# Three chained blocks in one kernel: new orders in the head and the first two stages, and the last block turned in groups of 96 tokens

## The reference

```python
def _attn_ref(q, k, v, g_norm):                 # [8, 8, 576, 64]
    kv = np.einsum('bhsd,bhse->bhde', k, v)
    out = np.einsum('bhsd,bhde->bhse', q, kv)
    rms = np.sqrt(np.mean(out * out, axis=-1, keepdims=True) + 1e-06)
    return out / rms * g_norm
# x = out as [4608, 512]
x = sigmoid(x @ w_gate) * (x @ w_val) @ w_out          # d_ff = 1536
x = silu(x @ w2_gate) * (x @ w2_val) @ w2_out
```

## Time and profile before

| what | us |
|---|---|
| median of 3 runs | 1748.52 (1748.45 to 1750.14) |
| the profiled execution | 1748.58 |
| its span, first to last instruction | 1745.8 |
| TensorE busy | 1721.4 (99%) |
| VectorE, ScalarE, GpSimd busy | 1205.7, 905.0, 377.6 |

### The profile page before, as it was taken

The page is one execution under the profiler, slowest core; times in us unless marked ns, Lnnn a source line. Parts: engine busy times, 40 slices in busy tenths (PEclk is TensorE's granted clock), DMA queues, the critical chain, the costliest instruction groups (busy, mean ns, idle before and its releaser), DMA issues.

```text
span 1745.8 us, 30864 instructions
## 1 busy us (share of the span) xinstructions
PE 1721.4 (99%) x11182; PEld 1689.5 (97%) x11182; DVE 1205.7 (69%) x1937; ACT 905.0 (52%) x1772; POOL 377.6 (22%) x326
## 2 busy tenths in 40 slices
PE   9999999999999999999999999999999999999998
PEld 7899899999999999999998999999999999999998
DVE  4977677787666678666679877787666668655555
ACT  5776676555444445444456555565444445444444
POOL 4722222013111125111126000013111125111111
PEclk9999999999999999999999999999999999999999
DMA  8786776576555566555555555566555566555553
GB/s 235 239 276 201 262 260 218 213 281 243 199 200 199 199 219 248 195 201 200 195 186 206 198 200 199 199 246 240 201 197 201 195 227 237 167 176 189 185 183 91
DMA packets 168982, 366.91 MB, mean 210 GB/s; under 512 B 12672, under 2 KB 128896, under 8 KB 168832
## 3 DMA queue, kind: packets, MB, share of 16 engines
q1 hardware_dynamic: 168832, 364.96, 61.1%
HBM read 234.36 MB, written 130.55 MB: 209 GB/s over the span
## 4 chain that ended last, share of the span: by engine, by line
PE 80%; DVE 2%; POOL 1%; issue 1%; ACT 0%; DVEq 0%; ACTq 0%; POOLq 0%
PE ps L833 78%; PE ps L775 1%; DVE arena L1398 0%; POOL arena L1650 0%; DVE arena L1380 0%; DVE wa L1236 0%; DVE hop L1330 0%; PE ps L694 0%; POOL wops L1595 0%; POOL wops L1594 0%; PE ps L674 0%; POOL wops L1592 0%; PE ps L707 0%; PE ps L681 0%; POOL wops L1597 0%
## 5 line engine op out<-in xcount | busy, mean ns | idle before, releaser
L833 PE MATMUL ps<-xo,wa 128*128 128x384 f32 x6048 | 1077.9, 336 | 6.2 <-ACT arena L1032 3.2
L833 PEld LDWEIGHTS ps<-xo,wa 128*128 128x128 f32 x6048 | 1047.3, 188 | 10.3 <-issue 4.0
L1032 ACT ACTIVATE arena<-ps 128x384 f32<-128x384 f32 x648 | 316.9, 491 | 566.9 <-PE ps L833 564.7
L1380 DVE TENSOR_TENSOR arena<-ps,arena 128x384 f32<-128x384 f32 x648 | 352.6, 553 | 361.6 <-PE ps L833 284.2
L833 PE MATMUL ps<-hop,wb 128*128 128x384 f32 x3024 | 538.1, 335 | 1.0 <-DVE arena L1398 0.7
L833 PEld LDWEIGHTS ps<-hop,wb 128*128 128x128 f32 x3024 | 522.9, 188 | 4.9 <-issue 1.7
L1650 POOL TENSOR_TENSOR arena<-arena 128x384 f32<-128x384 f32 x144 | 147.5, 1049 | 734.3 <-DVE arena L1380 734.3
L1330 DVE TENSOR_TENSOR hop<-arena,hop 128x384 fp32r<-128x384 f32 (+1 forms) x396 | 276.0, 719 | 34.1 <-ACT hop L1014 27.9
L1014 ACT ACTIVATE hop<-arena 128x384 fp32r<-128x384 f32 (+1 forms) x396 | 233.3, 609 | 63.4 <-DVE arena L1398 34.3
L1046 ACT ACTIVATE arena<-arena 128x384 f32<-128x384 f32 x216 | 112.7, 522 | 64.8 <-DVE arena L1380 64.7
L1398 DVE TENSOR_TENSOR arena<-arena 128x384 f32<-128x384 f32 x216 | 128.7, 597 | 20.3 <-DVE arena L1380 1.4
(11 more groups left out here) (76 smaller groups left out, 796.0 us busy)
## 6 DMA issues: line engine op xcount, KB each, us to landing
xo<-x_operands SPq DMA_DIRECT2D x168, 768.0 KB, 6.2
x_operands<-xo SPq DMA_DIRECT2D x84, 768.0 KB, 5.1
x<-arena SPq DMA_DIRECT2D x120, 384.0 KB, 3.2
arena<-x SPq DMA_DIRECT2D x96, 384.0 KB, 4.6
xraw<-x SPq DMA_DIRECT2D x22, 768.0 KB, 6.5
wops<-in_moe_w_gate_dram SPq DMA_DIRECT2D x24, 256.0 KB, 4.8
wops<-in_moe_w_val_dram SPq DMA_DIRECT2D x24, 256.0 KB, 4.2
wops<-in_moe_w_out_dram SPq DMA_DIRECT2D x48, 128.0 KB, 2.3
```

The source lines that it names most:

```text
L833: mm = pe.matmul(dst, lhsT, rhs, start=(pr in (1, 5, 2) and c == 0 and i == 0), stop=(c == 1 and i == 2), skip_group_check=(pr in (6, 7, 4 ...
L1032: nc.scalar.activation(dst, X(side), ACT.Copy).then_inc(copied, 1)
L1380: nc.vector.tensor_tensor(dst, acc, buf, ALU.add).then_inc(summed, 1)
```

## The change

Head: the order of calls is rewritten on all five engines. Fillers are left ahead of unit 0 alone, and two are put behind it. SP loads weight unit 0 right after unit 0, the gain after unit 2, weight unit 1 after unit 5. The o product of unit 8 and the transposes of unit 6 move into stage 0. GpSimd's differences are cut into two halves between which a power can stand. Stages 0 and 1: ScalarE, VectorE, SP and the steps of TensorE at which units 8 to 11 run are ordered anew; nothing else in them changes. End: a function of its own turns eight groups of 96 tokens; each goes out as one transfer, the fifth and seventh from ScalarE's queue, the others from SP's.

```diff
+        TURNS_END = BLK // SP_
+        o_stage_end = o_stage + [wflat[:, TURNS * DM:(TURNS + 1) * DM], att_o[:, 0:DM]]
-        ENDING = (3, 4, 5, 0, 1, 2)
-        END_BANK = {3: 6, 4: 7, 5: 2, 0: 3, 1: 0, 2: 1}
+        ENDING = (4, 5, 6, 7, 0, 1, 2, 3)
+        END_BANK = {4: 6, 5: 7, 6: 2, 7: 3, 0: 0, 1: 1, 2: 4, 3: 5}
+        SENT_BY_ACT = (4, 6)
-        FILLERS = {0: 4, 1: 4, 2: 4, 3: 2, 4: 1, 5: 1, 7: 1}
+        FILLERS = {0: 4}
-        KVQ_FIRST = ({5: 9, 15: 10}, {11: 11})
-        O_FIRST = ({7: 9}, {1: 10, 15: 11})
-        XT_FIRST = ({1: 7, 15: 8}, {9: 9, 22: 10})
+        KVQ_FIRST = ({5: 9, 17: 10}, {9: 11})
+        O_FIRST = ({1: 8, 7: 9, 21: 10}, {13: 11})
+        XT_FIRST = ({1: 6, 3: 7, 15: 8}, {7: 9, 21: 10})
 # SP, head
             load_unit(0)
+            load_w(0)
             load_unit(1)
+            load_unit(2)
             for d in (0, D):
                 sp.dma_start(g2[d:d + D, :], ...
-            load_w(0)
-            load_unit(2)
             load_unit(3)
             load_unit(4)
+            load_unit(5)
             load_w(1)
-            load_unit(5)
...
+            store_xo(0, 1)
+            store_xo(0, 2)
             load_unit(10)
-            store_xo(0, 1)
             store_xT(6)
+            load_w(4)
             store_xT(7)
-            store_xo(0, 2)
-            load_w(4)
-            store_xo(0, 5)
-            store_xT(8)
             load_w(5)
             load_unit(BETWEEN)
+            store_xT(8)
             load_xraw(1, 0)
+            load_unit(EARLY)
+            store_xo(0, 5)
+            store_xT(9)
...
 # TensorE, head
             unit_kv_qT(0)
+            keep_warm(att_bank(1))
+            keep_warm(att_bank(1))
+            unit_o(0)
             unit_kv_qT(1)
-            unit_o(0)
+            unit_kv_qT(2)
             unit_o(1)
-            unit_kv_qT(2)
             unit_xT(0)
...
             unit_kv_qT(5)
-            pe.wait_ge(xT_ready, 3)
-            for _ in range(2):
-                keep_warm(att_bank(6))
+            unit_kv_qT(6)
             unit_o(5)
             unit_xT(3)
-            unit_kv_qT(6)
+            unit_o(6)
+            unit_kv_qT(7)
             unit_xT(4)
-            unit_kv_qT(7)
-            unit_o(6)
-            pe.wait_ge(xT_ready, 5)
-            for _ in range(2):
-                keep_warm(att_bank(8))
             unit_o(7)
             unit_xT(5)
             unit_kv_qT(8)
-            pe.wait_ge(xT_ready, 6)
-            for _ in range(2):
-                keep_warm(att_bank(5))
-            unit_o(8)
-            unit_xT(6)
 # TensorE, end
+            def turn_end(i):
+                (waits as before, at groups 4, 6 and 0)
+                t, at = i // TC, i % TC * SP_
+                for d in range(KC):
+                    mm = pe.transpose(ps[0:SP_, END_BANK[i], d * P:(d + 1) * P],
+                                      res[:, t, d // 2, d % 2, at:at + SP_], ident[:])
+                mm.then_inc(turned, 1)
 # ScalarE, head
+            unit_kv_qT(0)
+            unit_sq(0)
+            split_w(0, RAW)
+            split_w(0, SUMMED)
+            unit_kv_qT(1)
+            unit_kv_qT(2)
+            unit_sq(1)
             act.wait_ge(g_loaded, 32)
-            unit_kv_qT(0)
-            unit_kv_qT(1)
-            unit_sq(0)
-            unit_sq(1)
-            split_w(0, RAW)
...
 # ScalarE, stage 0
             if g == 0:
+                unit_xT(6)
+                unit_sq(8)
                 unit_xT(7)
-                copy(1, 0)
                 split_w(2, SUMMED)
                 split_x(0, 5)
+                unit_kv_qT(9)
+                copy(1, 0)
+                split_x(0, 6)
                 copy(1, 1)
...
 # ScalarE, end
+            for e in SENT_BY_ACT:
+                act.wait_ge(o_copied, TURNS * (NB - 1) + e // 2 + 1)
+                nc.scalar.dma_start(end_rows(ENDING[e]), o_stage_end[ENDING[e]][0:SP_]).then_inc(end_stored, 16)
 # VectorE, head
             unit_norm(0)
+            split_w(0, RAW)
+            unit_scale(0)
+            split_w(0, SUMMED)
             unit_norm(1)
-            unit_scale(0)
-            split_w(0, RAW)
             unit_norm(2)
             unit_scale(1)
-            split_w(0, SUMMED)
 # VectorE, stage 0
                         x_s1_s3(0)
                         x_s2(0)
                         split_x(0, 5)
-                        total(11, 0)
+                        unit_scale(8)
                         split_x(0, 6)
-                        unit_scale(8)
                         x_s4(0)
                         unit_norm(9)
                         split_x(0, 7)
                         split_w(2, SUMMED)
+                        total(11, 0)
                         total(11, 1)
...
 # GpSimd
+            differences(0)
             rsqrt(0)
-            differences(0)
             rsqrt(1)
             rsqrt(2)
             differences(1)
-            for u in range(3, SHARED):
-                rsqrt(u)
+            rsqrt(3)
...
             differences(2)
+            differences_1_3(3)
             rsqrt(8)
-            differences(3)
+            differences_2_4(3)
             rsqrt(9)
             differences(4)
-            differences(5)
+            differences_1_3(5)
             rsqrt(10)
+            differences_2_4(5)
             rsqrt(11)
```

More of the change, by code:

```diff
@@ L501, in store_out @@
                     b, c, row = (at + first) // S, (at + first) % S // SP_, (at + first) % SP_
-                    sp.dma_start(out_dst[b, c, row:row + n], o_stage[i][first:first + n]
-                                 ).then_inc(out_stored[i % 2] if qq < QN - 1 else end_stored, 16)
+                    sp.dma_start(out_dst[b, c, row:row + n], o_stage[i][first:first + n]).then_inc(out_stored[i % 2], 16)
             load_unit(0)
+            load_w(0)
             load_unit(1)
+            load_unit(2)
             for d in (0, D):
                 sp.dma_start(g2[d:d + D, :], g_norm.rearrange("(d a) -> d a", a=1)).then_inc(g_loaded, 16)
-            load_w(0)
-            load_unit(2)
             load_unit(3)
             load_unit(4)
+            load_unit(5)
             load_w(1)
-            load_unit(5)
             load_unit(6)
@@ L648, in _ @@
                     store_xT(u)
-            for i in ENDING:
-                store_out(QN - 1, i)
+            for e, i in enumerate(ENDING):
+                if e in SENT_BY_ACT:
+                    continue
+                if e % 2 == 0:
+                    sp.wait_ge(o_copied, TURNS * (NB - 1) + e // 2 + 1)
+                else:
+                    sp.wait_ge(o_copied_end, e // 2 + 1)
+                sp.dma_start(end_rows(i), o_stage_end[i][0:SP_]).then_inc(end_stored, 16)
             for s in out_stored:
                 sp.wait_ge(s, 32 * HT * (NB - 1))
-            sp.wait_ge(end_stored, 32 * TURNS)
+            sp.wait_ge(end_stored, 16 * TURNS_END)
         @block.tensor
@@ L744, in _ @@
             unit_kv_qT(8)
-            pe.wait_ge(xT_ready, 6)
-            for _ in range(2):
-                keep_warm(att_bank(5))
-            unit_o(8)
-            unit_xT(6)
             def turn(qq, i):
                 n = TURNS * (qq - (QN - NB)) + i
[L754 to L772, removed]
+                if i == 0:
+                    pe.wait_ge(part_added, n_part(qq, 12, 1))
+                    pe.wait_ge(c21_done, 2 * qq + 2)
@@ L773, in turn @@
+                if n >= 2:
+                    pe.wait_ge(o_copied, n - 1)
                 t, at = i // HT, i % HT * P
                 for d in range(KC):
-                    mm = pe.transpose(ps[:, bank, d * P:(d + 1) * P], res[:, t, d // 2, d % 2, at:at + P], ident[:])
+                    mm = pe.transpose(ps[:, 6 + i % 2, d * P:(d + 1) * P], res[:, t, d // 2, d % 2, at:at + P], ident[:])
+                mm.then_inc(turned, 1)
+            def turn_end(i):
+                qq = QN - 1
+                if i == 4:
+                    pe.wait_ge(part_added, n_part(qq, 22, 1))
+                    pe.wait_ge(c21_done, 2 * qq + 2)
+                    pe.wait_ge(o_copied, TURNS * (NB - 1))
+                elif i == 6:
+                    pe.wait_ge(summed, n_summed(qq, 2, 11, 1))
+                elif i == 0:
+                    pe.wait_ge(part_added, n_part(qq, 11, 1))
+                    pe.wait_ge(summed, n_summed(qq, 2, 12, 1))
+                t, at = i // TC, i % TC * SP_
+                for d in range(KC):
+                    mm = pe.transpose(ps[0:SP_, END_BANK[i], d * P:(d + 1) * P], res[:, t, d // 2, d % 2, at:at + SP_],
+                                      ident[:])
@@ L854, in _ @@
             for i in ENDING:
-                turn(QN - 1, i)
+                turn_end(i)
         def w_operands(unit):
@@ L979, in _ @@
             split_x(0, 1)
-            unit_kv_qT(6)
-            unit_xT(4)
-            split_x(0, 2)
+            split_w(1, SUMMED)
             unit_kv_qT(7)
             unit_sq(6)
```

(16 more changed lines are left out.)

100 lines of the change are left out of this document (46 added, 54 removed).

## The result

The changed kernel takes 1754.88 us (median of 7, 1753.53 to 1757.63) against 1748.52 (median of 7 in the same series): ratio 1.0039, 95% interval 1.0028 to 1.0051. By the ratio it is slower by 6.8 us (interval 4.9 to 8.9). The profiled execution took 1757.63, the longest of the seven; its span is 1755.8, ten more than before. What follows is read from that one execution, so its terms sum to more than the medians differ by.

The account below looks back on a forecast made before the run. TensorE, busy for 99% of the span, was taken to bound the kernel, with VectorE tighter in stages 0 and 1. 1748.58 - 3.6 (head) - 1.4 (stages) - 1.4 (tail) = 1742.2, stated as 1742 us; range 1737.5 to 1751.

Parts of the forecast that it names:

- rival 1: Head: TensorE's clock stays low with few fillers, mark near 64, 12 us late, time 1758; chance 0.18.
- The head's step: Head, fillers removed and orders rewritten: it ends 3.6 us earlier; bounds nothing to 7.0.
- the mark: End of the head: VectorE's first sum of x quadrants, at 52.22 before, forecast at 48.6.
- The stores' step: Stages 0 and 1: SP's stores of operands and of x put behind loads, with no price of its own.
- Stages 0 and 1: Stretch from 52.2 to 94.7: the new order gains 1.4 us from VectorE's idle time; bounds 3.3 gained, 3 lost.
- The tail: End, eight groups of 96 tokens in fewer transfers: 1.4 us gained; bounds 2.6 gained, 0.5 lost.

Follow-up runs that it names:

- e6: Kernel before with all fillers behind unit 0's taken out, and the waits for `xT_ready` in which some stood; 1758.11 us, ratio 1.0050 to the kernel before.
- e9: Changed kernel with SP's five operand stores ahead of unit 12's load and fillers added ahead of units 2 and 5 only; 1747.56 us, ratio 0.9993 to the kernel before.
- e2: Changed kernel with SP's load of unit 12 moved behind the five operand stores; 1752.42 us, ratio 1.0013 to the kernel before.
- e3: Changed kernel with four fillers added ahead of unit 2's products; 1753.64 us, ratio 1.0014 to the kernel before.
- e4: Changed kernel with four fillers ahead of unit 2 and unit 12's load behind the five operand stores; 1749.31 us, ratio 0.9999 to the kernel before.
- e10: Changed kernel with fillers ahead of every unit from 2 to 8, operand stores still behind unit 12's load; 1748.90 us, ratio 0.9999 to the kernel before.
- e5: Changed kernel with fillers ahead of every unit from 2 to 8 and operand stores ahead of unit 12's load; 1746.02 us, ratio 0.9984 to the kernel before.
- e1: Kernel before with only its end taken from the change (eight groups of 96 tokens, eight transfers); 1748.21 us, ratio 0.9990 to the kernel before.
- e8: Changed kernel with operand stores ahead of unit 12's load and one row of ten fillers ahead of unit 5; 1753.19 us, ratio 1.0021 to the kernel before.
- e11: Changed kernel with operand stores first and thirteen fillers ahead of units 2, 3, 5, 7 and 8; 1748.70 us, ratio 0.9999 to the kernel before.

## Why the prediction was wrong

The time came out on the other side, by rival 1 and by one loss that no case had.

**The head's step failed.** Its term was 3.6 us earlier; in the profiled execution the mark came 9.2 later. It counted the fillers as TensorE time that can go, 12.0 us, and walked through the engines with every duration at full clock, since "once up it held with gaps of 0.7". In the old orders it held with those 12.0 us of fillers in and around the waits; e6 takes them out and loses 8.7 us. The walk was not bad while the clock was up: unit 1's loads (11.3 measured, 11.0 forecast for the last) and unit 2's v (13.5; its last load was forecast for 14.1). What it missed is that TensorE comes there early: unit 1 is done at 12.0 and not "near 13", so that there is a wait of 1.5 us where the forecast has nearly none, and it has no price for a wait ahead of small work.

**Rival 1 had the right effect with a wrong entrance.** I feared that the clock wouldn't rise before unit 3; it rose at 6.7 and fell again. The price was near: 6.1 us a unit forecast, 6.2 measured (1.55 + 1.22 + 2.19 + 1.22); but from 13.5 and not 9.6, for seven units: 54.0 for the first product against my 57.5, mark at 61.4 against 64. So its 1758 near the measured 1754.9 is partly luck: the time at half clock was forecast from another cause, and the stores' loss was not in it. It carried 0.18. The evidence for more was there: the only fall of the clock that the trace before showed ahead of its end came after an idle time, and the new order of loads made such idle times in the head likely, where the DMA share was 0.92. Against the rival I had set that TensorE would be busy without a break from 1.5 to 13; it had gaps of 0.7, 0.2 and 1.5 us by 13.5.
The Trainium skill (TensorE: Matmul & The Clock Gate, section "HAM oscillation — how this bites in real kernels") describes a kernel whose array is throttled again by each wait for DMA, where a burst of products is shorter than the wait behind it. The traces agree in kind and go further: here the waits ahead of a fall were 1.4 to 1.8 us, shorter than the work before them (3.0 us from 9.03 in the changed kernel), and e9's fall at 11.6 had none over 0.7.

**The stores' step was priced at nothing.** The prediction names "SP's stores of operands and of x put behind loads" and never asks what the load waits for. It waits for the end of the weights' splits, 10.6 us; the profile showed +5.2, the pairs of ratios 4.5 (changed kernel to e2), 2.6 (e3 to e4; 4.3 by their medians) and 2.6 (e10 to e5). The first of these is clear of noise, and so is the second by its medians.

**Stages 0 and 1** were right where the clock is up, in size and in mechanism: 1.4 forecast, 42.6 to 41.2 measured in e5, with VectorE busy for 39.3 us in both and its waits for ScalarE's copies gone. Why the changed kernel has 2.8 was not tested; its VectorE idles 1.1 us there and e5's 1.8. The lower bound of that term, 3 lost, doesn't follow from its own words: twice 4.4 idle us would be 4.4 more.

**The tail** was right: 1.4 forecast, 1.6 in the trace, 1.7 by e1's ratio (whose interval reaches zero). The 2.6 that the earlier last issue allowed did not come, at a DMA share of 0.96 to 1.01.

**Open:** whether the head's 3.6 us exist. No kernel ran the head at full clock without fillers, so the new orders were never seen free of both. Open are also what made the clock fall in e9 at 11.6, and e6's execution at 0.998.

## What to carry to other kernels

A filler may be more than waste to be counted: in these two kernels it held the clock. Before one is taken out, ask at each wait behind it how long TensorE idles and with what small work around it, and price the whole stretch to the next row of large products at half clock as one of the cases. In a queue written by hand, price a moved transfer by the longest wait ahead of it and by what bursts out behind it. Compare kernels of this kind by time and granted clock of each execution together.

## What the runs showed of the hardware

- TensorE at half clock stayed there through 40 us (13.5 to 53.9 in the changed kernel, 39.8 of them busy) of small products and transposes, 64 to 96 columns wide. In every head it came up only within a row of 128 x 256 or 128 x 384 products or some 2 us behind one (at 38.2 in e8, 57.8 in the changed kernel).
- It fell within 2.2 us of the end of a wait for a load of 1.4 to 1.8 us in seven heads (changed kernel, e2, e3, e4, e6, e8, e11). Shorter gaps also came ahead of falls: none over 0.7 in e9 at 11.6, two of 0.8 in e10 at 57.8, where it lasted 3.4 us. And a gap of 1.1 us did not make it fall in e5, e8, e10 and e11.
- The moment of the first rise is not the same in each execution: in the kernel before the unit 0 k-v product took 1.55 us and most of the second row of fillers ran at half clock; in e1, with the same head, the clock was up at 5.1 and down again for 6.8 us from 11.7.
- The spread of single times goes with the clock. Over 93 executions of the kernel before, half clock ranged from 3.5 to 28 us and the time from 1744.6 to 1757.5, correlation 0.90: up to 7 us of half clock the mean is 1747.2 (27 executions), from 21 to 28 us it is 1754.2 (19), some 0.4 us for each.
